# Storing both halves of the value product to DRAM and joining them on GpSimd by token group, in a fused attention and two-MLP kernel

## The chip, the cores and the metric

The kernel runs on one core of one Trainium2 chip. The metric is the device time of one execution in microseconds. A core has five engines that run their own instruction lists and meet only through semaphores: TensorE (PE, matrix products), VectorE (DVE), ScalarE (ACT), GpSimd (POOL) and SyncE (SP), which here issues every DMA. In the profile's rows "PEld" is TensorE loading the stationary operand, and "SPq" is the queue of SyncE.

## The reference

All inputs are float32. Three stages follow each other:

```python
def _attn_ref(q, k, v, s):                       # (4, 8, 576, 64); s is (4, 8, 576)
    scores = np.matmul(q, k.transpose(0, 1, 3, 2)) / np.sqrt(64)
    cum = np.cumsum(np.maximum(s, 0.0), axis=-1)
    bias = -(cum[:, :, :, None] - cum[:, :, None, :])
    scores = np.where(causal, -1e9, scores + np.minimum(bias, 0.0))
    attn = softmax(scores)
    return np.matmul(attn, v)
def _moe_ref(x, w_in, w_out, g_ln):              # x (2304, 512), hidden 1024
    h = x @ w_in
    solu = h * softmax(h)
    return (layer_norm(solu) * g_ln) @ w_out
def _moe2_ref(x, w1, w2, w3, w_out):             # hidden 768
    return np.maximum(np.maximum(x @ w1, x @ w2), x @ w3) @ w_out
```

The attention output of all 8 heads of a batch, side by side, is the row of 512 that enters the first MLP.

## The kernel before

**Precision.** Every product is made of float32 operands split in two: a high part that TensorE takes exactly, and a low part that holds the rest. A product is high times high plus the two mixed terms. In the value product the stationary operand `v_hl` (128 x 128) holds the high part of a head's v in columns 0 to 63 and the low part in columns 64 to 127. So the result in PSUM has 128 partitions for one head: partitions 0 to 63 are the product with the high half of v, partitions 64 to 127 that with the low half, and the two must be added to give the head's 64 output columns.

**Attention.** There are 32 heads (`HEADS`), worked on in slots. In slot t, TensorE (`slot`, L504) turns the probabilities of head t-1 (`turn`), computes the scores of head t, and does the value product of head t-2 (`values`) in two pieces: PV_A goes to PSUM bank 6 and PV_B to bank 7. The five engines each have their own slot function whose order is written out by hand, and each runs the steady slots two at a time in a loop (one turn is a pair, an even and an odd head), since all buffers come in twos.

- ACT (`slot`, L813 on): `pt_high` (copies turned probabilities, rounding them), `split_v`, five `exp`, and at the end of the slot `copy_vlo_a` and `copy_vlo_b`, which copy the low half (partitions 64 to 127) of banks 6 and 7 to SBUF.
- DVE: `q_low`, five `row_max`, four `pt_low`, and `add_a` and `add_b`, which add bank 6 or 7 (partitions 0 to 63) to the copied low half and write the result to `xT`, the attention output, that stays in SBUF.
- POOL: `qk_high` and `k_low` (the splits of q and k of head t+1: L670, L671, L672, L676), then `split_v` (L680, head t-1); in eight of the later pairs also a piece of the split of `w_in` (`split_win`, L691, L693).
- SP: `reload(t)`. All its waits stand in the queue, and everything behind a wait is held too:

```python
def reload(t, par, known=None):
    sp.wait_ge(k_hi_ready, t - 1); sp.wait_ge(q_lo_ready, t - 1); sp.wait_ge(k_lo_ready, t - 1)
    load_qk(t, par)
    if known != 2:
        sp.wait_ge(v_lo_ready, t - 2)
    load_v(t - 1, 1 - par)
    ...
    sp.wait_ge(scores_done, 3 * (t - 1))
    load_aux(t, par)
```

`load_qk` is two DMAs of 288 KB (L292), `load_v` two (L296, L297), `load_aux` one (L301). After every odd head of pairs 2 to 13 one piece of an MLP weight is loaded into `stage`: 512 KB of `w_in` in pairs 2 to 5 (L337), 256 KB of `w_out` in pairs 6 to 13 (L340).

**First MLP.** Tokens are taken in 6 groups of 384 (`GT`). For each group POOL's `divide(g)` (L723) multiplies a 128 x 1536 piece of `xT` by the reciprocals of the softmax sums, `rinvB`, which went through DRAM, and writes `xg`; ACT's `x_high` and DVE's `x_low` split it, and TensorE runs `hidden`, `turn_ln`, `second`. `divide(0)` stands in POOL's list between its slots 31 and 32, and ACT's first `x_high` stands before its slot 32, so the first group's input is prepared while the last heads are still in work. Later `divide`s stand ahead of the group before theirs. The second MLP follows.

## Time and profile before

| | |
|---|---|
| Median of 3 runs | 773.73 us (772.16 to 774.55) |
| Time of the profiled execution | 776.48 us |
| Span of the profiled execution, first to last instruction | 774.2 us |
| Busy share of the span | PE 93%, DVE 54%, ACT 42%, POOL 29% |
| Mean granted TensorE clock | 0.989 of full speed |
| DMA | 45.26 MB; HBM read 39.43 MB, written 5.38 MB |

The attention stage takes the first 240 us of the span. There all engines are busy; in the two MLPs behind it TensorE is busy nearly all the time and the others are not. Busy shares of a whole span are therefore no guide to a change in the attention stage: the rows further down are read stretch by stretch. A busy TensorE is a modelled figure, and an idle engine costs only where something waits for it.

### The profile page before, as it was taken

How to read it: one execution, taken by the hardware profiler on the slowest of the kernel's cores; microseconds unless marked ns; L12 is line 12 of the kernel's file. 1: busy time of each engine (PE TensorE's matmuls, PEld its weight loads, DVE VectorE, ACT ScalarE, POOL GpSimd, SP SyncE). 2: the span in 40 equal slices, each digit the busy share in tenths (PEclk: the TensorE clock that was granted, in tenths of full speed). 3: DMA queues.
4: the chain of work that ended last, by engine and by line, in shares of the span. 5: the costliest groups of instructions: out<-in, count | busy, mean ns of one | idle time of the engine just before them, and what ended most of it. 6: DMA issues, size and time to landing. Idle time of an engine off the chain costs nothing.

```text
span 774.2 us, 12663 instructions
## 1 busy us (share of the span) xinstructions
PE 720.6 (93%) x4248; PEld 664.9 (86%) x4248; DVE 418.0 (54%) x766; ACT 328.5 (42%) x795; POOL 226.3 (29%) x242
## 2 busy tenths in 40 slices
PE   2798898999889899999999999999999999999997
PEld 1787787888777788889898989999989999899995
DVE  8799999999995684635354463612313213132120
ACT  1688788888874443414232242412112112121111
POOL 6665768989742641304040200000000000000000
PEclk9799999999999999999999999999999999999999
DMA  6555455555341101105200022000010010000101
GB/s 136 118 140 153 130 144 131 141 133 137 95 91 42 42 13 29 42 1 145 60 0 0 0 81 83 1 14 28 1 41 1 1 40 1 30 11 0 41 0 41
DMA packets 46579, 45.26 MB, mean 58 GB/s; under 512 B 22164, under 2 KB 37652, under 8 KB 46516
## 3 DMA queue, kind: packets, MB, share of 16 engines
q1 hardware_dynamic: 46548, 44.86, 21.9%
q8 instruction: 18, 0.29, 0.2%
q14 instruction: 13, 0.11, 0.1%
HBM read 39.43 MB, written 5.38 MB: 58 GB/s over the span
## 4 chain that ended last, share of the span: by engine, by line
PE 65%; DVE 10%; DMA 7%; issue 6%; POOL 5%; SPq 4%; ACT 2%; DVEq 0%; POOLq 0%; ACTq 0%
PE ps L606 10%; PE ps L605 10%; PE ps L604 10%; DMA qk_raw<-in_qk_dram 7%; PE ps L536 4%; PE ps L538 4%; PE ps L537 4%; PE ps L524 3%; PE ps L526 3%; PE ps L525 3%; PE ps L617 3%; PE ps L619 3%; PE ps L618 3%; DVE nmax L1007 2%; POOL qk_b L676 2%
## 5 line engine op out<-in xcount | busy, mean ns | idle before, releaser
L606 PE MATMUL ps<-x_lo,w_hi 128*128 (+1 forms) x432 | 144.4, 334 | 0.0
L604 PE MATMUL ps<-x_hi,w_hi 128*128 128x384 f32 x432 | 144.3, 334 | 0.0
L605 PE MATMUL ps<-x_hi,w_lo 128*128 128x384 f32 x432 | 144.3, 334 | 0.0
L788 ACT ACTIVATE probs<-ps,nmax 128x576 f32<-128x576 f32 (+4 forms) x160 | 82.6, 530 | 17.2 <-DVE nmax L1007 17.2
L798 ACT ACTIVATE pt_hi<-ps 128x512 fp32r<-128x512 f32 (+1 forms) x128 | 69.8, 569 | 34.5 <-PE ps L433 28.3
L433 PE MATMUL ps<-ident,probs 128*128 128x128 f32 x480 | 74.3, 286 | 10.4 <-DVE pt_lo L1014 5.8
L440 PE MATMUL ps<-pt_hi,v_hl 128*128 128x256 f32 (+2 forms) x256 | 67.7, 294 | 16.5 <-DVE xT L1034 13.6
L604 PEld LDWEIGHTS ps<-x_hi,w_hi 128*128 128x128 f32 x432 | 81.1, 188 | 0.2
L605 PEld LDWEIGHTS ps<-x_hi,w_lo 128*128 128x128 f32 x432 | 81.1, 188 | 0.2
L606 PEld LDWEIGHTS ps<-x_lo,w_hi 128*128 128x128 f32 x432 | 81.1, 188 | 0.0
L1014 DVE TENSOR_TENSOR pt_lo<-ps,pt_hi 128x512 fp32r<-128x512 f32 (+1 forms) x128 | 78.0, 649 | 4.8 <-ACT pt_hi L798 3.9
L415 PE MATMUL ps<-k_a,q_a 128*128 128x288 f32 (+2 forms) x192 | 64.3, 342 | 14.5 <-DVE rinvT L1052 14.1
L1007 DVE TENSOR_REDUCE nmax<-ps 128x1 f32<-128x576 f32 (+4 forms) x160 | 72.7, 484 | 4.6 <-PE ps L420 3.2
L933 ACT ACTIVATE m_hi<-stage 128x384 fp32r<-128x384 f32 x36 | 18.9, 525 | 124.9 <-DVE stage L1193 124.9
L440 PEld LDWEIGHTS ps<-pt_hi,v_hl 128*128 128x128 f32 x256 | 49.3, 193 | 21.9 <-issue 14.3
L536 PE MATMUL ps<-lnT_hi,wout_hi 128*128 128x384 f32 x192 | 64.4, 335 | 2.7 <-DVE lnT_lo L1138 2.7
L433 PEld LDWEIGHTS ps<-ident,probs 128*128 128x128 f32 x480 | 53.3, 145 | 15.8 <-issue 6.9
L1195 DVE TENSOR_TENSOR m_lo<-stage,m_hi 128x384 fp32r<-128x384 f32 x36 | 20.1, 558 | 82.2 <-ACT m_hi L933 82.2
L538 PE MATMUL ps<-lnT_lo,wout_hi 128*128 128x384 f32 x192 | 64.2, 335 | 0.0
L537 PE MATMUL ps<-lnT_hi,wout_lo 128*128 128x384 f32 x192 | 64.2, 334 | 0.0
L441 PE MATMUL ps<-pt_lo,v_hl 128*128 128x256 f32 (+2 forms) x256 | 61.0, 286 | 0.0
L524 PE MATMUL ps<-win_hi,x_hi 128*128 128x512 f32 x144 | 57.5, 399 | 2.8 <-DVE ln L1122 2.1
(102 smaller groups left out, 1441.5 us busy)
## 6 DMA issues: line engine op xcount, KB each, us to landing
qk_raw<-in_qk_dram SPq DMA_DIRECT2D x64, 288.0 KB, 4.2
rinvB<-rsum_dram SPq DMA_DIRECT2D x24, 192.0 KB, 3.8
stage<-in_moe_w_dram SPq DMA_DIRECT2D x18, 256.0 KB, 4.4
out_dram<-stage SPq DMA_DIRECT2D x18, 256.0 KB, 2.0
v_raw<-in_v_dram SPq DMA_DIRECT2D x32, 128.0 KB, 2.4
stage<-in_moe_w_out_dram SPq DMA_DIRECT2D x14, 256.0 KB, 2.7
stage<-in_moe_w_in_dram SPq DMA_DIRECT2D x4, 512.0 KB, 3.6
aux_dram<-setup SPq DMA_DIRECT2D x1, 576.0 KB, 4.5
```

The costliest lines, as they stand in the source:

```text
L433: mm = pe.transpose(ps[:, GBANK[g], P * n:P * (n + 1)], probs[1 - par][:, o:o + P], ident[:, :])
L440: pe.matmul(dst, v_hl[par][:, j, :], pt_hi[par][:, a0:a1], start=(n == 0), stop=False)
L524: pe.matmul(dst, x_hi[ab][:, c, :], win_hi[:, c, cols], start=(c == 0), stop=False)
L536: pe.matmul(dst, wout_hi[:, f, cols], lnT_hi[:, f, :], start=(f == 0), stop=False)
L537: pe.matmul(dst, wout_lo[:, f, cols], lnT_hi[:, f, :], start=False, stop=False)
L538: mm = pe.matmul(dst, wout_hi[:, f, cols], lnT_lo[:, f, :], start=False, stop=(f == FB - 1))
L604: pe.matmul(dst, w_hi[f][:, i, c, :], x2_hi[par][:, c, :], start=(c == 0), stop=False)
L605: pe.matmul(dst, w_lo[f][:, i, c, :], x2_hi[par][:, c, :], start=False, stop=False)
L606: mm = pe.matmul(dst, w_hi[f][:, i, c, :], x2_lo[:, c, bass.ds(g * GT, GT)], start=False, stop=(c == KC - 1))
L788: act.activation(dst, SCORES[c], ACT.Exp, bias=nmax[par][:, c:c + 1], accum_out=sums_all[:, c, bass.ds(t, 1)]).then_inc(exp_done, 1)
L1007: dve.tensor_reduce(nmax[par][:, c:c + 1], SCORES[c], AX_XY if c == NCH - 1 else AX_X, ALU.max, negate=True).then_inc(max_done, 1)
L1014: dve.tensor_tensor(pt_lo[1 - par][:, o:o + n], ps[:, GBANK[g], 0:n], f32(pt_hi[1 - par][:, o:o + n]), ALU.subtract).then_inc(pt_lo_done, 1)
```

## The change

What the attention stage makes of a head's value product is changed:

- **Removed**: ACT's two copies of 64 partitions (`copy_vlo_a`, `copy_vlo_b`), and DVE's two adds (`add_a`, `add_b`) with the semaphores that TensorE, ACT and POOL wait on for them.
- **Added on ACT**: one copy of all 128 partitions of both banks (288 columns of each, 128 x 576) to one of two `halves` buffers.
- **Added on SP**: `store_x`, one DMA of 288 KB for each head, from `halves` to a DRAM tensor `x_dram` (head, partition, position). In the steady loop it stands behind `load_aux` in every `reload`, so ahead of the weight load and of the next head's q and k. `load_xa(b)` reads the high half of one batch (8 heads) back into `xT` with two DMAs of 576 KB; `load_xb(g)` reads the low half of one token group into a new buffer `xb` with four DMAs of 192 KB. The first of these stand among the last heads' reloads.
- **Added on POOL**: in each `divide(g)` an add of 128 x 1536, `xT` plus `xb`, ahead of the multiplication.
- **Moved**: the boundary between the pieces of the value product, so that each bank holds 288 columns. PV_A had pieces of 320, 256 and 128 columns and has 288, 224 and 96; PV_B had 4 of 256 and one of 128 and has 3 of 288, one of 256 and one of 128. The sum of columns and the number of matmuls stay.

```diff
-    PV_A = [(0, J0 + PAD, J0 + 3 * P, 0), (1, J1, J1 + 2 * P, PAD), (2, J2, J2 + P, PAD + P)]
+    PV_A = [(0, J0 + PAD, J0 + PAD + HALF, 0), (1, J1, J1 + HALF - PAD, PAD), (2, J2, J2 + HALF - P - PAD, P + PAD)]
...
+    x_dram = nc.dram_tensor("x_dram", (HEADS, P, S), F32, kind="Internal").ap()
...
@@ SP, reload @@
                 load_aux(t, par)
+                if known is None or known >= 5:
+                    store_x(t - 5, 1 - par)
+
+            def store_x(h, par):
+                sp.wait_ge(x_copied, h + 1)
+                rows = x_dram[bass.ds(h, 1)].rearrange("a p s -> (a p) s")
+                sp.dma_start(rows, halves[par][:, :, :].rearrange("p a b -> p (a b)")).then_inc(x_stored[par], 16)
+
+            def load_xa(b):
+                for par in range(2):
+                    sp.wait_ge(x_stored[par], 16 * (b + 1) * HB // 2)
+                for par in range(2):
+                    src = x_dram[HB * b:HB * (b + 1), 0:D, :].rearrange("(j r) d s -> r d j s", r=2)[par]
+                    sp.dma_start(xT[D * par:D * (par + 1), :, S * b:S * (b + 1)], src).then_inc(xa_loaded, 16)
...
@@ SP, last heads @@
             reload(HEADS - 4, 0)
+            load_xa(0)
             reload(HEADS - 3, 1)
+            load_xb(0)
             reload(HEADS - 2, 0)
+            load_xa(1)
             sp.wait_ge(rinv_done, 1)
...
@@ TensorE, slot @@
                     if known != 2:
-                        pe.wait_ge(xa_done, t - 2)
+                        pe.wait_ge(x_copied, t - 2)
                     values(t, par, 6, PV_A)
...
@@ POOL, divide @@
+                cols = xT[:, :, bass.ds(g * GT, GT)]
+                pool.wait_ge(xb_loaded, 64 * (g + 1))
+                pool.tensor_tensor(cols, cols, xb[:, :, :], ALU.add).then_inc(x_added, 1)
                 pool.wait_ge(rinvB_loaded, 64 * (g + 1))
                 if known != 0:
                     pool.wait_ge(x_lo_ready, 3 * g)
-                pool.tensor_tensor(xg[:, :, :], xT[:, :, bass.ds(g * GT, GT)], rinvB[:, :, :], ALU.mult).then_inc(xg_ready, 1)
+                pool.wait_ge(x_added, g + 1)
+                pool.tensor_tensor(xg[:, :, :], cols, rinvB[:, :, :], ALU.mult).then_inc(xg_ready, 1)
...
@@ ACT, end of a slot @@
-                act.activation(vlo_a[:, :], ps[D:P, 6, 0:QA], ACT.Copy).then_inc(vloa_copied, 1)
-                act.activation(vlo_b[:, :], ps[D:P, 7, 0:QB], ACT.Copy).then_inc(vlob_copied, 1)
+                if known is None or known >= 4:
+                    act.wait_ge(x_stored[par], (t - 2 - par) * 8)
+                act.wait_ge(pv_done, 2 * (t - 2) + 2)
+                act.activation(halves[par][:, :, :], ps[:, 6:8, 0:HALF], ACT.Copy).then_inc(x_copied, 1)
...
@@ DVE, slot @@
-                if live(known, 3):
-                    add_a(t, par, known)
...
-                if live(known, 3):
-                    add_b(t, par, known)
```

On SP, at the end of a turn of the loop over pairs 6 to 13, behind the odd head's `load_aux` (L301), the list changes so (in the rows "ISA" and REGISTER_ALU compute addresses and wait counts, and the next turn begins with the even head's `load_qk`):

```order
 L301 DMA qk_b1<-aux_dram 4x1152
-L340 ISA x2
-L340 DMA stage<-in_moe_w_out_dram 128x512
-L338 REGISTER_ALU
-L338 COMPARE_AND_BRANCH
+L331 REGISTER_ALU
+L333 ISA
+L333 DMA x_dram<-halves0 128x576
+L373 ISA x2
+L373 DMA stage<-in_moe_w_out_dram 128x512
+L371 REGISTER_ALU
+L371 COMPARE_AND_BRANCH
```

The store of a head now stands ahead of the weight load, and both stand ahead of the next pair's q and k.

On SP, at the reloads of heads 28 to 30, straight behind that loop (xT and xb are the buffers for the high and the low half):

```order
 L301 DMA qk_b0<-aux_dram 4x1152
+L333 DMA x_dram<-halves1 128x576
+L341 DMA xT<-x_dram 64x4x576 x2
 L292 DMA qk_raw1<-in_qk_dram 64x1152 x2
 L296 DMA v_raw0<-in_v_dram 64x64
 L297 DMA v_raw0<-in_v_dram 128x4x64
 L301 DMA qk_b1<-aux_dram 4x1152
+L333 DMA x_dram<-halves0 128x576
+L352 DMA xb<-x_dram 64x4x192 x4
 L292 DMA qk_raw0<-in_qk_dram 64x1152 x2
```

Ahead of head 29's q and k now stand a store and the read of a whole batch's high halves, and ahead of head 30's a store and four reads of low halves.

On POOL, where the attention stage hands over to the first MLP, the list of the changed kernel reads as follows (L722 is the split of v, L764 the add, L769 the multiplication that was L723, L795 the scaling of `w_out`):

```order
L764 TENSOR_TENSOR xT<-xT,xb 128x4x384
L769 TENSOR_TENSOR xg<-xT,rinvB 128x1536
L722 TENSOR_TENSOR v_hl<-v_raw,v_hl 128x5x64
L764 TENSOR_TENSOR xT<-xT,xb 128x4x384
L769 TENSOR_TENSOR xg<-xT,rinvB 128x1536
L795 TENSOR_SCALAR wout_hi<-stage,g_sb 128x512 x8
```

Each multiplication has an add ahead of it now; the order of the others has not moved.

## Rows read from the trace of the kernel before

**Rows 1.** Windows: busy us of each engine, then clock, DMA share, GB/s

```profile
40.00:60.00 20.00, 18.30 (x142) 16.68 (x141) 19.25 (x37) 17.73 (x53) 12.66 (x15) 1.00 0.60 159
160.00:180.00 20.00, 18.55 (x144) 16.85 (x142) 19.59 (x39) 17.61 (x53) 18.36 (x20) 1.00 0.52 138
```

**Rows 2.** Waits from 40 to 230 us: us in total, times, longest

```profile
POOL q_a L670 <- DMA qk_raw<-in_qk_dram: 25.5, 12, 3.9
...
PE ps L440 <- DVE xT L1034: 13.4, 21, 1.6
```

**Rows 3.** Groups by shape, 40 to 250 us: busy, mean ns, idle before

```profile
L788 ACT ACTIVATE probs<-ps,nmax 128x576 f32<-128x576 f32 x28 | 20.6, 735 | 1.0 <-DVE nmax L1007 1.0
...
L805 ACT ACTIVATE vlo_a<-ps 64x320 f32<-64x320 f32 x31 | 13.5, 434 | 6.8 <-PE ps L441 6.1
...
L1034 DVE TENSOR_TENSOR xT<-ps,vlo_a 64x320 f32 x24 | 11.6, 484 | 0.7
L812 ACT ACTIVATE vlo_b<-ps 64x256 f32<-64x256 f32 x31 | 11.5, 369 | 1.2 <-PE ps L441 1.2
...
L1041 DVE TENSOR_TENSOR xT<-ps,vlo_b 64x256 f32 x24 | 9.9, 413 | 0.4
```

**Rows 4.** Timeline of POOL in one pair: start us, us, what, idle before

```profile
130.66 0.67 POOL L670 TENSOR_SCALAR q_a<-qk_raw 128x576 fp32r<-128x576 f32 x1 [1.24 <-DMA qk_raw<-in_qk_dram]
...
132.57 1.92 POOL L676 TENSOR_TENSOR qk_b<-qk_raw,k_a 64x576 fp32r<-64x576 f32 x1
134.45 0.87 POOL L680 TENSOR_TENSOR v_hl<-v_raw,v_hl 128x320 fp32r<-128x320 f32 x1
...
143.74 0.67 POOL L670 TENSOR_SCALAR q_a<-qk_raw 128x576 fp32r<-128x576 f32 x1 [1.33 <-DMA qk_raw<-in_qk_dram]
```

**Rows 5.** Timeline of SP's queue in the same pair

```profile
135.49 0.47 SPq L296 DMA_DIRECT2D v_raw<-in_v_dram  x1
136.14 0.45 SPq L297 DMA_DIRECT2D v_raw<-in_v_dram  x1
136.84 0.27 SPq L301 DMA_DIRECT2D qk_b<-aux_dram  x1
137.43 0.36 SPq L340 DMA_DIRECT2D stage<-in_moe_w_out_dram  x1
138.49 1.18 SPq L292 DMA_DIRECT2D qk_raw<-in_qk_dram  x2
```

**Rows 6.** Chain in order of time: last q/k load of two pairs

```profile
85.58 5.29 DMA qk_raw<-in_qk_dram
...
139.20 4.28 DMA qk_raw<-in_qk_dram
```

**Rows 7.** Timeline of SP's queue, the pair that loads 512 KB

```profile
83.62 0.36 SPq L337 DMA_DIRECT2D stage<-in_moe_w_in_dram  x1
```

**Rows 8.** Timeline of POOL: splits of heads 4, 28, 29 and 30

```profile
32.92 0.67 POOL L670 TENSOR_SCALAR q_a<-qk_raw 128x576 fp32r<-128x576 f32 x1 [1.45 <-PE ps L420]
...
195.68 0.67 POOL L670 TENSOR_SCALAR q_a<-qk_raw 128x576 fp32r<-128x576 f32 x1 [0.95 <-DMA qk_raw<-in_qk_dram]
202.88 0.67 POOL L670 TENSOR_SCALAR q_a<-qk_raw 128x576 fp32r<-128x576 f32 x1
208.76 0.67 POOL L670 TENSOR_SCALAR q_a<-qk_raw 128x576 fp32r<-128x576 f32 x1 [0.43 <-PE ps L420]
```

**Rows 9.** Timeline of SP's queue: q and k of heads 29, 30

```profile
196.42 1.11 SPq L292 DMA_DIRECT2D qk_raw<-in_qk_dram  x2
...
202.15 1.11 SPq L292 DMA_DIRECT2D qk_raw<-in_qk_dram  x2
```

**Rows 10.** Waits of PE from 200 to 242 us

```profile
PE ps L440 <- DVE xT L1034: 2.8, 4, 1.5
```

**Rows 11.** Timeline of POOL and ACT at the hand-over

```profile
230.58 0.88 POOL L680 TENSOR_TENSOR v_hl<-v_raw,v_hl 128x320 fp32r<-128x320 f32 x1 [4.83 <-ACT v_hl L778]
231.41 3.49 POOL L723 TENSOR_TENSOR xg<-xT,rinvB 128x1536 f32<-128x1536 f32 x1
...
235.69 0.62 ACT L857 ACTIVATE x_hi<-xg 128x512 fp32r<-128x512 f32 x1
236.33 0.60 ACT L798 ACTIVATE pt_hi<-ps 128x512 fp32r<-128x512 f32 x1
```

**Rows 12.** Waits of POOL from 240 to 440 us

```profile
POOL xg L723 <- DVE x_lo L1091: 82.5, 5, 22.7
```

More of the change, by code:

```diff
@@ L124, in attention_and_mlp @@
             nmax = [sb(a, f"nmax{i}", [P, NCH]) for i in range(2)]
-            vlo_a = sb(a, "vlo_a", [D, QA])
-            vlo_b = sb(a, "vlo_b", [D, QB])
+            halves = [sb(a, f"halves{i}", [P, 2, HALF]) for i in range(2)]
             q_a = [sb(a, f"q_a{i}", [P, SP], F32R) for i in range(2)]
@@ L207, in attention_and_mlp @@
         pv_done = sem("pv_done")
-        vloa_copied = sem("vloa_copied")
-        vlob_copied = sem("vlob_copied")
-        xa_done = sem("xa_done")
-        xb_done = sem("xb_done")
+        x_copied = sem("x_copied")
+        x_stored = [sem(f"x_stored{i}") for i in range(2)]
+        xa_loaded = sem("xa_loaded")
+        xb_loaded = sem("xb_loaded")
+        x_added = sem("x_added")
         sums_turned = sem("sums_turned")
@@ L325, in reload, with load_xb, reload_pair, load_win @@
                 load_aux(t, par)
-            reload(2, 0, 2)
-            reload(3, 1)
-            def reload_pair(pair):
-                reload(2 * pair, 0)
-                reload(2 * pair + 1, 1)
-            with sp.Fori(2, 2 + KC) as pair:
+                if known is None or known >= 5:
[10 more added lines that the diff above has]
+                    sp.dma_start(xT[D * par:D * (par + 1), :, S * b:S * (b + 1)], src).then_inc(xa_loaded, 16)
+            def load_xb(g):
+                if g > 0:
+                    sp.wait_ge(x_added, g)
+                for part in range(2):
+                    b_, s0 = divmod(g * GT + part * GT // 2, S)
+                    for par in range(2):
+                        src = x_dram[HB * b_:HB * (b_ + 1), D:P, s0:s0 + GT // 2].rearrange("(j r) d t -> r d j t", r=2)[par]
+                        dst = xb[D * par:D * (par + 1), :, part * GT // 2:(part + 1) * GT // 2]
+                        sp.dma_start(dst, src).then_inc(xb_loaded, 16)
+            reload(2, 0, 2)
+            reload(3, 1, 3)
+            def reload_pair(pair, known=None):
+                reload(2 * pair, 0, known)
+                reload(2 * pair + 1, 1, known and known + 1)
+            def load_win(pair):
+                sp.dma_start(stage[:, bass.ds(pair * FF - 2 * FF, FF)], w_in[bass.ds(pair * P - 2 * P, P), :]).then_inc(w_loaded, 16)
+            reload_pair(2, 4)
+            load_win(2)
+            with sp.Fori(3, 2 + KC) as pair:
                 reload_pair(pair)
-                sp.dma_start(stage[:, bass.ds(pair * FF - 2 * FF, FF)], w_in[bass.ds(pair * P - 2 * P, P), :]).then_inc(w_loaded, 16)
+                load_win(pair)
             with sp.Fori(2 + KC, 2 + KC + FB) as pair:
@@ L377, in _ @@
                 load_rinv(g)
+                load_xb(g)
             def stage_block(f, slot):
@@ L573, in _ @@
             hidden(1, 1, 0)
-            pe.wait_ge(xa_done, HEADS)
-            pe.wait_ge(xb_done, HEADS)
+            pe.wait_ge(x_copied, HEADS)
             pe.wait_ge(rinvT_ready, 4)
@@ L1023, in invert_sums @@
                 dve.reciprocal(flat, flat).then_inc(rinv_done, 1)
-            def columns(t, par, known):
-                pair = (t - 4 + par) // 2 if known is not None else (t - 4 + par) >> 1
-                return (pair % KC) * TOKENS + (pair // KC) * S
-            def add_a(t, par, known):
-                flat = xT[:, :, :].rearrange("p c t -> p (c t)")
-                dve.wait_ge(vloa_copied, t - 2)
-                dve.tensor_tensor(flat[D * (1 - par):D * (2 - par), bass.ds(columns(t, par, known), QA)], ps[0:D, 6, 0:QA],
-                                  vlo_a[:, :], ALU.add).then_inc(xa_done, 1)
-            def add_b(t, par, known):
-                flat = xT[:, :, :].rearrange("p c t -> p (c t)")
-                dve.wait_ge(vlob_copied, t - 2)
-                dve.tensor_tensor(flat[D * (1 - par):D * (2 - par), bass.ds(columns(t, par, known) + QA, QB)], ps[0:D, 7, 0:QB],
-                                  vlo_b[:, :], ALU.add).then_inc(xb_done, 1)
             q_low(0, 0)
```

39 lines of the change are left out of this document (17 added, 22 removed).

## The prediction, written before the changed kernel was run

> **What bounds the kernel now.** I first read the windows of the attention stage. The reader is to see that DVE is busy 19.25 of 20 us early in the stage and 19.59 of 20 us later, ACT 17.7, TensorE 18.5 by its modelled figure [rows 1]. Taken alone that says DVE is the bound, and a change that takes work from DVE must win. The waits say something else beside it. TensorE waits 13.4 us in all, 21 times, for DVE's `add_a` before it may start PV_A. But POOL also waits 25.5 us, 12 times, for the q and k of the next head to land [rows 2]. Twelve is once in nearly every pair, always ahead of an even head.
>
> So I followed that wait around one pair in the timelines. POOL begins an even head's splits at 130.66 us, on the landing of the load. They and the split of v behind them end at 134.45 + 0.87 = 135.32 us [rows 4]. SP was waiting for exactly that: its next issue starts at 135.49, and it goes on without a gap through v, v, aux and the weight piece to the two q/k loads at 138.49 [rows 5]. The chain of waits then runs through the second of these loads, from 139.20 for 4.28 us, to 143.48 [rows 6], and POOL begins the next even head at 143.74, having sat idle for 1.33 us [rows 4]. This is a closed ring, POOL to SP to DMA to POOL, of 13.08 us, with no slack at any step, and it is as long as the pair. The kernel is thus held by two things at once: DVE's list (97% full) and this ring. Shortening the first gains nothing if the second gets longer.
>
> **The change part by part.**
>
> *DVE loses two adds*, 484 + 413 = 897 ns a head [rows 3], 1.8 us a pair. If DVE alone set the pace, 32 heads would gain up to 29 us. ACT and TensorE leave less room: ACT is busy 17.61 of 20 us, so at 88% of its present time it is full [rows 1]. What TensorE could get back is the 13.4 us it now waits for the adds [rows 2].
>
> *ACT* replaces copies of 434 + 369 = 803 ns [rows 3] by one of 128 x 576 from PSUM. The nearest row is the exponential of that shape, 735 ns [rows 3]. I take 735 ns, a gain of 0.07 us a slot that lies beside the ring: zero. The bounds are 0 and 2 us over the stage. The first copy could run while TensorE was still in PV_B and the new one can not, but ACT's next work needs TensorE's next transposes, so what is queued behind it would wait anyway.
>
> *TensorE* keeps its columns and its number of matmuls: zero. Its new wait at PV_A is for the copy at the end of the slot before, about 3 us earlier: zero. If that copy itself waits for the store that frees its buffer, everything moves; the store is issued one slot before the copy that needs the buffer, and I count 4 us between landing and need.
>
> *SP and the queue, 12 pairs.* From head 5 on each `reload` issues a store of 288 KB, behind aux and ahead of the weight load and q/k. For the ring this is the odd head's store: one store per turn. Its price is bounded from below by its issue alone. The v and aux issues follow each other by 0.65 to 0.70 us [rows 5], so 0.65 us. From above it is bounded by its bytes, since the queue drains in order. The trace has that experiment. With 256 KB of weights ahead of q/k, the time from the weight issue to the landing is 143.48 - 137.43 = 6.05 us [rows 5, 6]. With 512 KB it is 85.58 + 5.29 - 83.62 = 7.25 us [rows 6, 7]. So 256 KB more cost 1.20 us, and 288 KB would cost 1.35 us. The mean rate agrees roughly: 138 GB/s at a share of 0.52 is 265 GB/s when busy [rows 1], 1.1 us for the store. I take 1.2 us, between the two and near the measured one. The intervals it applies to are those between even heads 4 and 28, from 32.92 to 195.68 us [rows 8], 12 of them: 12 x 1.2 = **14.4 us** (7.8 to 16.2).
>
> The page "DMA: Bandwidth & Descriptors", section "Anatomy of one DMA", of the Trainium skill prices moving bytes at 436 GB/s on top of a fixed cost. By it the store would hold the queue 0.68 us, the issue would be its dearer part, and this term would be about 8 us instead of 14.4. The row with 256 KB more disagrees with the page by a factor of two, and I go by the row.
>
> *SP and the queue, last heads.* Ahead of head 29's q/k come a store and 1152 KB of high halves, ahead of head 30's a store and 768 KB of low halves: 2496 KB in all. Together with what stands there already (two times 576 KB, 144 and 18 KB) it is 3810 KB, 14.7 us at 265 GB/s. From the issue at 196.42 [rows 9] with about 1.5 us of latency this ends at 212.6 us. POOL began head 30 at 208.76, and it waited for TensorE there, not for DMA [rows 8]. That is 3.8 us late, and head 29 alone gives the same size: POOL began it without waiting at 202.88 [rows 8]. The two overlap. The read of batch 1 behind them runs while SP waits for the reciprocals anyway. I take **4 us** (0 if the queue's idle time takes it all; 8 if both add).
>
> *POOL's add at the hand-over.* `divide(0)` ran at 231.41 for 3.49 us, straight behind the split of v [rows 11]. The add has the same shape and two operands in SBUF: 3.49 us, ahead of it. ACT's first `x_high` at 235.69 needs the result, and ACT's last transposed probabilities at 236.33 are queued behind it [rows 11]. With `xg` at 238.4 instead of 234.9, ACT would start at about 238.5: **+2.7 us** (0 to 3.5), and TensorE's last slot and the first MLP tile wait for ACT. The five later adds (17.5 us of POOL) stand ahead of a wait of 82.5 us in five times that POOL has there [rows 12]: zero.
>
> *What the relief of DVE still gives.* Outside the 12 intervals, from 200 to 242 us, TensorE waits 2.8 us for the adds [rows 10]: **-2 us** (-3 to 0).
>
> The sum is 14.4 + 4 + 2.7 - 2 = **+19.1 us**. The profiled execution took 776.5 us, with 774.2 us of span; that becomes 795.6. The median of the runs shown is 2.8 us below the profiled one, so the time is 792.8, rounded 793 us.
>
> **The rivals.**
>
> *A, the relief wins (faster).* If the store's issue and bytes vanish in the ring's idle time, the pace is set by DVE, ACT and TensorE, and the 13.4 us of waits go, less 2.7 us at the hand-over: 773.7 - 10.7 = 763 us. Against it speaks that the ring has no idle step. It decides if the ring shortens by more than the 0.65 us that the issue alone costs. POOL's step is the one that could: `k_low` takes 1.92 us there [rows 4]. The page "SBUF — State Buffer" of the Trainium skill, section "Who interferes with whom", says that a DVE instruction with at most one SBUF input does not contend with GpSimd. The adds have one, so by that rule their removal leaves `k_low` as long as it is. Without that rule I would still doubt A, since the ring waits for DMA 1.33 us, not for POOL alone. Chance 0.17.
>
> *B, a draw.* The price is the bare issue, 7.8 us, the last heads' loads are hidden, and the relief gives back 8 to 10 us wherever the ring is not last. 774 us within 2. Chance 0.08.
>
> *C, the queue is worse (slower still).* The store's writes cost twice the 1.35 us, or the bulk reads add up to 8 us and TensorE's idle time brings its clock down. The clock is 1.00 in the stretches shown [rows 1], so a drop would be new. 14.4 doubles and 4 becomes 8: 773.7 + 37.5 = 811 us. Chance 0.13.
>
> *The forecast*, the ring grows by a store per turn: 0.62, its own range 779 to 802 (the sum with all lower bounds is 7.8 + 0 + 0 - 3 = +4.8; with all upper ones +27.7).
>
> **How the numbers follow.** Runs of this kernel can tell about 0.3%, 2.3 us, from no change. Faster: A, 0.17, and a little of B, 0.18. Same: 0.08. Slower: the forecast and C less what B takes, 0.74. The range leaves out half of A and the upper part of C: 765 to 804 us.
>
> **What the changed profile would show.** If I am right, the even heads' first split on POOL comes every 14.2 to 14.4 us where weight pieces of 256 KB are loaded, with idle time of 1.3 us or more ahead of it that ends on the q/k DMA. DVE's busy time falls from 19.6 to about 15.5 of 20 us. The wait of PV_A for DVE is gone, and TensorE waits for splits (`k_low`, `q_low`) or scores instead. The row of the store's issue is followed 0.65 us later by the weight issue, and the landing of the q/k loads is 7.2 us or more behind the store's issue. Around the reloads of heads 29 and 30 POOL waits 3 to 5 us for DMA. ACT sits idle about 2.7 us before its first `x_high`. If pairs take 13 us or less, the ring was not what I took it for and A holds. If ACT waits for the store to free `halves`, or TensorE for `x_copied`, I missed a wait.

## The result, and the profile after

The changed kernel takes 797.81 us (median of 4 runs, 793.96 to 800.65) against 773.69 us (4 runs, 772.16 to 774.55): ratio 1.0311, 95% interval 1.0264 to 1.0357. It is slower by 24 us, where the prediction said 19, in a range that holds it. A second comparison, on another chip, gave 794.67 against 774.44 us, ratio 1.0245 (1.0221 to 1.0268). The direction is sure; the size is between 19 and 24 us.

The profiled execution of the changed kernel took 800.65 us. The head of its page, for the busy shares, the granted clock in 40 slices, and the bytes:

```profile
span 798.9 us, 12576 instructions
...
PE 727.7 (91%) x4248; PEld 672.2 (84%) x4248; DVE 398.5 (50%) x702; ACT 325.1 (41%) x763; POOL 249.3 (31%) x248
...
PEclk9799999999987998999999999999999999999999
...
HBM read 48.87 MB, written 14.82 MB: 80 GB/s over the span
```

The reader is to see the low digits of the clock, 8 and 7 where the attention stage hands over to the first MLP (220 to 260 us) and 8 once more from 300 us, and 19 MB more of traffic. The windows of the attention stage, with the columns of [rows 1]:

```profile
40.00:60.00 20.00, 19.27 (x150) 17.37 (x149) 18.36 (x33) 18.16 (x54) 13.39 (x15) 1.00 0.68 196
160.00:180.00 20.00, 17.54 (x135) 15.89 (x134) 16.52 (x30) 16.95 (x47) 15.59 (x17) 1.00 0.64 173
```

From 160 to 180 us every engine is less busy than before: DVE has fallen from 19.59 to 16.52 us, TensorE from 18.55 to 17.54. Nobody is full any more; something that is no engine sets the pace. The waits from 40 to 250 us:

```profile
POOL q_a L712 <- DMA qk_raw<-in_qk_dram: 41.4, 14, 4.7
PEld ps L478 <- DVE pt_lo L1049: 38.4, 50, 5.0
DVE q_a L1035 <- POOL q_a L712: 31.8, 20, 5.9
```

TensorE's wait for the adds is gone, and POOL's wait for q and k has grown from 25.5 us in 12 times [rows 2] (the same 25.5 if its window too is taken to 250 us) to 41.4 in 14. DVE, which waited 2.7 us for POOL before, now waits 31.8. Its `pt_lo` stands behind that work in its list, so TensorE now waits for `pt_lo`: 30.8 us by its own row, 3.0 before. One turn of the ring, in SP's queue and on POOL (compare [rows 4, 5]):

```profile
139.11 0.47 SPq L296 DMA_DIRECT2D v_raw<-in_v_dram  x1
139.77 0.44 SPq L297 DMA_DIRECT2D v_raw<-in_v_dram  x1
140.48 0.27 SPq L301 DMA_DIRECT2D qk_b<-aux_dram  x1
141.00 0.36 SPq L333 DMA_DIRECT2D x_dram<-halves  x1
141.69 0.35 SPq L373 DMA_DIRECT2D stage<-in_moe_w_out_dram  x1
142.63 1.15 SPq L292 DMA_DIRECT2D qk_raw<-in_qk_dram  x2
```

```profile
134.29 0.67 POOL L712 TENSOR_SCALAR q_a<-qk_raw 128x576 fp32r<-128x576 f32 x1 [2.14 <-DMA qk_raw<-in_qk_dram]
...
138.08 0.87 POOL L722 TENSOR_TENSOR v_hl<-v_raw,v_hl 128x320 fp32r<-128x320 f32 x1
...
148.20 0.67 POOL L712 TENSOR_SCALAR q_a<-qk_raw 128x576 fp32r<-128x576 f32 x1 [2.17 <-DMA qk_raw<-in_qk_dram]
```

and the load in the chain of work that ended last:

```profile
143.24 4.69 DMA qk_raw<-in_qk_dram
```

The ring is closed as before, POOL to SP to DMA to POOL, and takes 148.20 - 134.29 = 13.91 us where it took 13.08. The 0.83 us come apart: from the first issue of v to the weight issue 2.58 us against 1.94, which is +0.64 us for one more issue, and from the weight issue to the landing of q and k 6.24 us against 6.05, +0.19. POOL's step is 4.82 against 4.83 us.

At the hand-over, POOL and ACT (compare [rows 11]):

```profile
244.11 0.88 POOL L722 TENSOR_TENSOR v_hl<-v_raw,v_hl 128x320 fp32r<-128x320 f32 x1 [6.60 <-ACT v_hl L821]
244.94 3.47 POOL L764 TENSOR_TENSOR xT<-xT,xb 128x1536 f32<-128x1536 f32 x1
248.56 3.43 POOL L769 TENSOR_TENSOR xg<-xT,rinvB 128x1536 f32<-128x1536 f32 x1
```

```profile
252.11 0.63 ACT L892 ACTIVATE x_hi<-xg 128x512 fp32r<-128x512 f32 x1 [3.46 <-POOL xg L769]
252.64 0.58 ACT L841 ACTIVATE pt_hi<-ps 128x512 fp32r<-128x512 f32 x1
```

To place the loss I cut the execution at five events that both kernels have: POOL's first split of heads 4, 28 and 31, the third and the sixth `x_low` of DVE (L1091 before, L1103 after), and the end of the span. Microseconds of each stretch:

| stretch | before | after | after, second comparison | cost |
|---|---|---|---|---|
| head 4 to head 28, 12 turns | 162.8 | 170.0 | 169.0 | +6.2 to 7.3 |
| head 28 to head 31 | 25.4 | 29.7 | 29.0 | +3.6 to 4.3 |
| head 31 to third `x_low` | 28.5 | 34.8 | 33.8 | +5.3 to 6.2 |
| third to sixth `x_low` | 33.9 | 37.6 | 37.4 | +3.5 to 3.7 |
| sixth `x_low` to the end | 490.7 | 493.6 | 492.7 | +2.0 to 2.9 |

With head 4 0.2 us later in the first run, and 0.7 us earlier in the second, the costs sum to 24.7 and 19.8 us of span. I read the stretches rather than the totals, and they repeat unequally. Each kernel has one trace, the changed one two. The fourth stretch repeats within 0.5 us over all kernels below with the same order, and the third within 0.1 us over the five that keep the hand-over of before. The first does not: two variants whose SP list is the changed kernel's up to head 28 took 168.2 and 172.3 us in it. Most of that scatter lies in its first four turns (58.7 to 61.7 us); the last eight took 109.0 to 110.8 us in these four traces, against 104.6 in the one trace of the kernel before. So the late turns are the safer measure of the ring: 0.55 to 0.78 us each. The end scatters by 1.8 us even where its code is unchanged (see the account further down).

The fourth stretch had no term in the prediction. DVE and POOL there:

```profile
285.91 0.68 DVE L1103 TENSOR_TENSOR x_lo<-xg,x_hi 128x512 fp32r<-128x512 f32 x1
287.31 0.15 DVE L1145 TENSOR_SCALAR stats<-stats 128x1 f32<-128x1 f32 x1 [0.71 <-ACT e L905]
287.38 9.35 DVE L1117 SCALAR_TENSOR_TENSOR wout_lo<-stage,g_sb,wout_hi 128x512 fp32r<-128x512 f32 x8
```

```profile
288.74 2.95 POOL L779 TENSOR_SCALAR ln<-ln,stats 128x1024 f32<-128x1024 f32 x1 [0.21 <-POOL stats L776]
291.65 3.87 POOL L764 TENSOR_TENSOR xT<-xT,xb 128x1536 f32<-128x1536 f32 x1
```

`wout_lo` is the split of the second weight of the first MLP, eight instructions of 128 x 512. It took 6.17 us in the trace of before and takes 9.35 us here, beside the third group's new add. The rows of its eight instructions (shortest, median and longest in ns), before and after, say how:

```profile
L1105 DVE SCALAR_TENSOR_TENSOR wout_lo<-stage,g_sb,wout_hi x8: 739/744/1530, 269.4 to 274.8; 128x512 fp32r<-128x512 f32 x8
L1117 DVE SCALAR_TENSOR_TENSOR wout_lo<-stage,g_sb,wout_hi x8: 741/742/3924, 287.4 to 296.0; 128x512 fp32r<-128x512 f32 x8
```

The eight are not all slower. The median is the same 0.74 us, and one of them takes 3.92 us, about as long as POOL's whole add.

### The profile page after: what moved, and what is told of

Its sections match the earlier page's. It is cut to its first block, busy times and chain, and to the rows that moved or that the text cites. A ratio compares the mean times of both kernels' runs of the same rounds, so it can differ in the third digit from the quotient of the medians.

```text
span 798.9 us, 12576 instructions
## 1 busy us (share of the span) xinstructions
PE 727.7 (91%) x4248; PEld 672.2 (84%) x4248; DVE 398.5 (50%) x702; ACT 325.1 (41%) x763; POOL 249.3 (31%) x248
## 4 chain that ended last, share of the span: by engine, by line
PE 65%; DMA 9%; POOL 7%; DVE 6%; issue 6%; SPq 5%; ACT 2%; POOLq 0%; DVEq 0%; ACTq 0%
PE ps L646 9%; PE ps L648 9%; PE ps L647 9%; DMA qk_raw<-in_qk_dram 9%; PE ps L579 4%; PE ps L581 4%; PE ps L580 4%; PE ps L567 3%; PE ps L568 3%; PE ps L569 3%; PE ps L659 3%; PE ps L661 3%; PE ps L660 3%; POOL qk_b L718 2%; PE ps L478 2%
## 5 line engine op out<-in xcount | busy, mean ns | idle before, releaser
L478 PE MATMUL ps<-ident,probs 128*128 128x128 f32 x480 | 80.0, 295 | 40.6 <-DVE pt_lo L1049 37.7
L478 PEld LDWEIGHTS ps<-ident,probs 128*128 128x128 f32 x480 | 55.0, 149 | 49.6 <-DVE pt_lo L1049 45.7
L1042 DVE TENSOR_REDUCE nmax<-ps 128x1 f32<-128x576 f32 (+4 forms) x160 | 69.7, 482 | 6.8 <-PE ps L465 5.7
L485 PE MATMUL ps<-pt_hi,v_hl 128*128 128x288 f32 (+4 forms) x256 | 70.7, 301 | 0.0
L486 PE MATMUL ps<-pt_lo,v_hl 128*128 128x288 f32 (+4 forms) x256 | 64.1, 296 | 0.0
L1035 DVE SCALAR_TENSOR_TENSOR q_a<-qk_raw,q_a 64x576 fp32r<-64x576 f32 x32 | 40.6, 1268 | 35.0 <-POOL q_a L712 34.7
```

What stands on the lines that cost most here:

```text
L478: mm = pe.transpose(ps[:, GBANK[g], P * n:P * (n + 1)], probs[1 - par][:, o:o + P], ident[:, :])
L485: pe.matmul(dst, v_hl[par][:, j, :], pt_hi[par][:, a0:a1], start=(n == 0), stop=False)
```

## The experiments

All ratios are to the kernel before on the same chip, with a 95% interval. The single moves were compared on other chips than the two results above, and the changed kernel's own ratio is 1.0311 or 1.0245. A variant's total is therefore weak evidence of what one move is worth; the stretches are better.

**Store behind q and k** (changed kernel; the store of a head comes one reload later, straight behind the issue of the next q and k):

```diff
                 load_qk(t, par)
+                if known is None or known >= 6:
+                    store_x(t - 6, par)
...
                 load_aux(t, par)
-                if known is None or known >= 5:
-                    store_x(t - 5, 1 - par)
```

> The changed kernel with each store issued one reload later, straight behind the load of q and k instead of ahead of the weight load and the next q and k. Same DMAs, same bytes. Theory R (the store's place in the ring POOL to SP to DMA to POOL is what costs): with 256 KB weight pieces the even heads' first split on POOL comes every 13.0 to 13.2 us again instead of 13.8 to 13.9, and the kernel gains 7 to 10 us on the changed one, to 788 to 791 us. Rival (the queue's bytes cost, wherever the store stands): the interval stays at 13.8 us and the time within 2 us of 798 us.

Measured: 787.23 us, ratio 1.0138 (1.0110 to 1.0167). Head 4 to head 28 took 164.8 us, so 5.2 of the 7.3 us came back. The late turns took 13.0 to 13.5 us (one 14.1), not 13.0 to 13.2 as expected. A new wait took some of it, since the buffer is now freed later (waits from 40 to 230 us):

```profile
ACT halves L849 <- DMA x_dram<-halves: 11.5, 6, 3.8
```

The store's place in SP's list is what cost the ring. This leaves open whether its issue or its bytes do.

**Few bytes, same issues** (changed kernel; leaves out of the stores all but 16 partitions, and the reads repeat stored rows, so the output isn't the reference's):

```diff
-                sp.dma_start(rows, halves[par][...]).then_inc(x_stored[par], 16)
+                sp.dma_start(rows[0:16, :], halves[par][0:16, ...]).then_inc(x_stored[par], 16)
```

> The changed kernel with stores of 16 partitions instead of 128 (36 KB instead of 288 KB), in the same place; the reads from DRAM keep their size but read rows that were stored, so the attention output is not the reference's. It splits the store's price in the ring into issue and bytes. If the issue on SP is the price (0.68 us between neighbours), the interval of even heads with 256 KB weights stays at 13.7 us, 0.1 below the changed kernel's, and the time falls by 2 us at most. If the bytes are the price as predicted (1.2 us or more), the interval returns to 13.1 to 13.3 us and the time falls by 6 to 8 us.

Measured: 796.76 us, ratio 1.0264 (1.0234 to 1.0294), no faster than the changed kernel. Late turns take 13.5 to 13.9 us, and the last eight sum to 110.8 us, as with full stores. An eighth of the store's bytes gives the same ring. So the store's bytes cost nothing that shows there, and what is left of the store is its issue.

**A store alone, in the kernel before** (a copy of 288 KB from `xT` to a spare DRAM tensor, in the place of `store_x`; first from head 5 on, then from head 6 on):

```diff
                 load_aux(t, par)
+                if known is None or known >= 6:      # 5 in the first version
+                    sp.wait_ge(xa_done, 2)
+                    sp.wait_ge(xb_done, 2)
+                    rows = x_dram[bass.ds(t - 5, 1)].rearrange("a p s -> (a p) s")
+                    sp.dma_start(rows, xT[:, 0, 0:S]).then_inc(x_stored, 16)
```

> The kernel before, its copies and adds on DVE kept, with one extra store of 288 KB per head from head 5 on, in the place where the changed kernel has it (the data stored are two heads' finished output, and nothing reads them). Theory R: the store alone costs 0.85 us or more in each of 12 even-to-even intervals, 10 to 16 us in all, so 784 to 790 us, and since DVE keeps its adds here the first four intervals, where DVE's relief hid it in the changed kernel, are longer too. Rival (the relief of DVE gave nothing, the ring alone counts): the same +7.5 us up to head 28 as in the changed kernel, so 781 us.

Measured: 790.38 us, ratio 1.0179 (1.0150 to 1.0207). This is not the price of a store. The turn from head 4 to head 6 alone took 21.5 us, since the first copy waited on SP for an add of a slot later; the late turns took 13.6 to 14.1. With the first copy moved by one head:

> The kernel before with an extra store of 288 KB per head in the changed kernel's place, from head 6 on. In the run of that kind from head 5 on, the first store waited for an add of one slot later, and the interval of heads 4 to 6 was 21.5 us; this one takes that wait out. Theory: with 256 KB weights each even-to-even interval is 13.75 us as there, 0.75 above the kernel before; the interval of heads 4 to 6 falls to 16 to 17 us; in all 8 to 11 us more than the kernel before up to head 28, and a ratio to it of 1.011 to 1.015. Then what DVE's relief gave back in the changed kernel's loop is 1 to 3 us. Rival: the ratio stays at 1.018, and the relief is worth 6 us or more.

Measured: 777.79 us, ratio 1.0077 (1.0046 to 1.0109). The last eight turns take 13.56 to 13.94 us, 109.9 in all against 104.6 in the kernel before: +0.67 us a turn (110.8 in the changed kernel). With ACT, DVE and POOL doing exactly their old work, the store alone makes the late turns of the changed kernel. So the longer turn there is no effect of the copies, the adds or the banks. In all it cost less than expected (a ratio of 1.011 to 1.015 was): the first four turns took 57.5 us, no more than before, and head 28 to head 31 23.0 us against 25.4, on which more below.

**A load in that place** (kernel before; 288 KB of q and k read into a spare buffer instead of the store, from head 5 on):

```diff
+                if known is None or known >= 5:
+                    if known != 5:
+                        sp.wait_ge(x_stored, 16 * (t - 5))
+                    sp.dma_start(spare_in[:, :], qkT[bass.ds(t - 5, 1)].rearrange("a d i s -> (a d i) s")).then_inc(x_stored, 16)
```

> The kernel before, with an extra load of 288 KB for each head from head 5 on (head t-5's q and k, 128 rows of 576, into a buffer nobody reads), in the place where the changed kernel has its store; all of the computation stays. Each load waits for the one before it, which was issued a slot earlier. The run with a store in that place gave intervals of mostly 13.5 to 13.9 us between even heads, h28 to h31 23.0 us, and a ratio of 1.0077. Theory 1, only the issue on SP counts (0.65 us), whichever way the bytes go: intervals of 13.6 to 13.9 us again, ratio 1.005 to 1.011. Theory 2, the bytes of a load compete with q and k and those of a store don't (the row of 512 KB against 256 KB of weights, 1.20 us for 256 KB, compared loads): 0.65 us for the issue and up to 1.35 us for the bytes, intervals of 14.2 to 14.8 us and a ratio of 1.014 to 1.025, with the landing of q and k 0.6 us or more farther behind their issue than in the run with the store.

Measured: 783.18 us, ratio 1.0086 (1.0064 to 1.0108), the ratio of the store within its interval. The last eight turns sum to 111.9 us, 0.24 a turn more than with a store, and one of them is 14.92. So in the late turns a load's bytes may cost a little, a fifth of the 1.35 us that my upper bound gave them. Theory 2 falls there. The first four turns, with weight pieces of 512 KB, took 61.1 us against 57.5 with a store; since the changed kernel's own scatter by 3 us, that settles nothing.

**Weight pieces behind the even head's q and k** (changed kernel):

```diff
-                reload_pair(pair)
-                load_wout(pair)
+                reload_pair(pair, None, lambda: load_wout(pair))   # issued behind load_qk of the even head
```

> The changed kernel with each weight piece loaded behind the even head's q and k instead of ahead of them; the stores stay in their place. Theory R (issues and bytes ahead of the even load set the ring): the ring loses a weight issue (0.63 to 0.95 us) and its bytes, so the even intervals fall from 13.8 to 12.7 to 13.1 us, and the 512 KB ones by more; 12 intervals give 9 to 14 us, a ratio of 1.013 to 1.020. Rival (with the adds gone another engine sets the pace at 13.8 us, or the odd ring becomes as long): the intervals stay at 13.5 us or more and the ratio at 1.027 to 1.031.

Measured: 782.29 us, ratio 1.0134 (1.0096 to 1.0171). The last eight turns take 12.6 to 13.2 us, all twelve 154.7 us: 15.3 us less than in the changed kernel and 8.1 less than before. SP's queue there, with nothing between the store and q and k:

```profile
135.02 0.28 SPq L301 DMA_DIRECT2D qk_b<-aux_dram  x1
135.56 0.37 SPq L335 DMA_DIRECT2D x_dram<-halves  x1
136.19 1.14 SPq L292 DMA_DIRECT2D qk_raw<-in_qk_dram  x2
```

**The same move in the kernel before:**

> The kernel before with the weight pieces loaded behind the even head's q and k, all else unchanged. It tells what held the kernel before at 13.0 us a pair. If both the ring and DVE's list, as I read the profile: the ring gets 0.8 us shorter, DVE's list at 97% allows 0.1 to 0.3 us of it in the later pairs and up to 0.8 us in the first ones, 2 to 6 us in all, a ratio of 0.992 to 0.997. Rival (the ring alone): 12.3 us a pair, 8 us or more, a ratio below 0.990.

Measured: 773.18 us, ratio 0.9979 (0.9961 to 0.9997). That is a little less than expected, and far from the rival. The twelve turns sum to 160.5 us against 162.8, but the gain lies in the first four; the last eight take 106.0 us, not less than the 104.6 of before. The window says what holds them:

```profile
100.00:120.00 20.00, 18.08 (x138) 16.27 (x138) 19.54 (x37) 17.73 (x53) 13.37 (x16) 1.00 0.52 127
```

DVE is busy 19.54 of 20 us. The two belong together: with the adds DVE's list holds the late turns at a mean of 13.1 us and more though the ring is shorter, without them the mean is 12.8, but only if the ring is shortened first. With the weights moved in both kernels, the change gains 160.5 - 154.7 = 5.8 us over the twelve turns in spite of its store, 106.0 - 102.6 = 3.4 of it in the last eight. This is the relief that rival A spoke of, and the change as made can't collect it.

**The bulk reads spread** (changed kernel; the reads of the first two batches and of the first group's low halves stand piece by piece behind the q and k of heads 20 to 25):

```diff
+            pieces = [lambda: load_xa(0, (0,)), lambda: load_xa(0, (1,)), lambda: load_xb(0, (0,)),
+                      lambda: load_xb(0, (1,)), lambda: load_xa(1, (0,)), lambda: load_xa(1, (1,))]
...
-            load_xa(0)
...
-            load_xb(0)
...
-            load_xa(1)
```

> The changed kernel with the reads of batches 0 and 1 (high halves) and of group 0 (low halves) taken out of the last heads' reloads and spread, one piece of 384 to 576 KB behind each load of q and k, over heads 20 to 25. Theory: heads 29 to 31 no longer wait for them; the stretch from head 28's split to head 31's falls from 29.7 us to about the 25.4 us of the kernel before plus a store or two, 26 us, and the kernel gains 3 to 5 us, a ratio to the kernel before of 1.025 to 1.027. Rival: they cost the same wherever they stand (the queue's bytes), heads 20 to 28 get longer by as much, and the ratio stays at 1.031.

Measured: 788.03 us, ratio 1.0196 (1.0155 to 1.0237). Head 28 to head 31 takes 22.4 us, 7.3 less than in the changed kernel and 3.0 less than before, and head 4 to head 28 took 168.7 us, no longer than the 169.0 and 170.0 of the changed kernel. So the rival falls: spread out behind the loads of q and k, the same bytes cost nothing that shows. The gain is more than the 3 to 5 us expected, since 25.4 us is no floor: with a store alone the kernel before takes 23.0 us there. Where the reads stood, SP's queue of the changed kernel reads:

```profile
203.23 0.35 SPq L333 DMA_DIRECT2D x_dram<-halves  x1
203.68 1.34 SPq L341 DMA_DIRECT2D xT<-x_dram  x2
205.13 1.19 SPq L292 DMA_DIRECT2D qk_raw<-in_qk_dram  x2
...
209.49 0.35 SPq L333 DMA_DIRECT2D x_dram<-halves  x1
209.88 2.61 SPq L352 DMA_DIRECT2D xb<-x_dram  x4
212.60 1.35 SPq L292 DMA_DIRECT2D qk_raw<-in_qk_dram  x2
```

and the chain has, for the load issued at 205.13:

```profile
205.72 9.02 DMA qk_raw<-in_qk_dram
```

The reads hold the queue by their issues (1.34 and 2.61 us), and here by their bytes too: this q and k took 9.02 us to land against 4.69 in the ring. 1152 KB directly ahead do what 288 KB two issues ahead do not. The read of batch 1 does the same to head 31. Its q and k, before and after:

```profile
216.11 1.12 SPq L292 DMA_DIRECT2D qk_raw<-in_qk_dram  x2
221.09 0.67 POOL L670 TENSOR_SCALAR q_a<-qk_raw 128x576 fp32r<-128x576 f32 x1 [1.29 <-DMA qk_raw<-in_qk_dram]
```

```profile
221.69 1.30 SPq L341 DMA_DIRECT2D xT<-x_dram  x2
225.34 1.13 SPq L292 DMA_DIRECT2D qk_raw<-in_qk_dram  x2
232.87 0.67 POOL L712 TENSOR_SCALAR q_a<-qk_raw 128x576 fp32r<-128x576 f32 x1 [3.27 <-DMA qk_raw<-in_qk_dram]
```

From the issue to POOL's split it is 5.0 us before and 7.5 us after.

**The first group's add one slot earlier on POOL** (changed kernel, ahead of its slot 31):

```diff
+            join(0)              # the wait for xb and the add
             slot(HEADS - 1, 1, HEADS - 1)
             divide(0, 0)         # now the multiplication alone
```

> The changed kernel with POOL's first add moved ahead of its slot 31, where it idles 6.6 us. Theory: ACT's idle time of 3.5 us before its first x_high is the add's, so the gap from the split of v of head 30 to x_high falls from 8.0 to 4.5 us, TensorE keeps its full clock at the first tile, and the kernel gains 3 to 5 us on the changed one, to 793 to 795 us. Rival (the data from DRAM come late there, not the add): the add waits for its loads in the new place, holds up the split of v of head 30, and the time stays within 1 us of 798 us.

Measured: 794.88 us, ratio 1.0240 (1.0212 to 1.0267). The total can't be told from the second comparison of the changed kernel. The stretch can: from head 31 to the third `x_low` 28.7 us, against 34.8 and 33.8 with the add in its place (32.5 to 33.8 in the other five variants that keep it there) and 28.5 before. The add at the hand-over costs 4 to 6 us, all of that stretch's loss but 0.2. TensorE's clock there did not stay full as expected: 0.91 from 236 to 256 us.

**The third group's add behind `wout_lo`** (changed kernel):

```diff
                 cols = xT[:, :, bass.ds(g * GT, GT)]
+                if isinstance(g, int) and g == 2:
+                    pool.wait_ge(wout_lo_ready, 1)
```

> The changed kernel with POOL's add for group 2 waiting until DVE has made wout_lo. Theory (an add on POOL and wout_lo on DVE, both with two operands in SBUF, hold each other up): DVE's wout_lo falls from 9.35 us back to 6.2 us, and the kernel gains 3 to 4 us, a ratio of 1.026 to 1.028. Rival: wout_lo is longer for another reason (the normalization at its side), stays above 9 us, and the ratio stays at 1.031.

Measured: 789.10 us, ratio 1.0207 (1.0168 to 1.0247). The split of the weight on DVE, and POOL's add behind it:

```profile
283.51 6.17 DVE L1119 SCALAR_TENSOR_TENSOR wout_lo<-stage,g_sb,wout_hi 128x512 fp32r<-128x512 f32 x8
```

```profile
289.84 3.46 POOL L766 TENSOR_TENSOR xT<-xT,xb 128x1536 f32<-128x1536 f32 x1 [2.02 <-DVE wout_lo L1119]
```

6.17 us again, and the add 3.46 us instead of 3.87. Third to sixth `x_low` takes 33.99 us, as before. In all seven kernels with the add beside `wout_lo` (both runs of the changed one and the five variants with that order) this stretch took 37.4 to 37.8 us; in the seven without the collision 33.8 to 34.0. The clock shows the rest of it; windows from 296 to 316 us, of the changed kernel and of this one:

```profile
296.00:316.00 20.00, 17.48 (x82) 16.19 (x83) 12.49 (x26) 8.01 (x14) 6.97 (x5) 0.83 0.24 54
```

```profile
296.00:316.00 20.00, 20.00 (x110) 18.99 (x109) 11.50 (x25) 7.59 (x13) 9.19 (x8) 1.00 0.36 79
```

**The changed kernel again**, for a closer interval and a second trace:

> The changed kernel itself, unchanged, on the chip of the two others and in more rounds, as the base for the differences: a ratio of 1.025 to 1.033. If it is below 1.025, the gains of the single moves are smaller than their differences to 1.0311 say.

Measured: 794.67 us, ratio 1.0245 (1.0221 to 1.0268), with the stretches shown in the table. It lies just below the 1.025 set beforehand, so the condition holds: by their ratios the single moves gain less than their differences to 1.0311 say. Against 1.0245 they are 8.6 us (weights), 3.8 (reads), 0.4 (first add) and 2.9 (third group's add).

**All four moves together** (changed kernel; weights behind q and k, reads spread, both adds moved; nothing left out):

> The changed kernel with four moves together, nothing left out: weight pieces behind the even head's q and k (alone it gave a ratio of 1.0134), the reads of batches 0 and 1 and of group 0's low halves spread over heads 20 to 25 (1.0196 alone), the first add ahead of POOL's slot 31 (1.024 alone), the add for group 2 behind wout_lo (1.0207 alone), against 1.0311 for the changed kernel. Theory: the costs are separate places on one chain, so the gains of 14, 7, 5 and 3 to 4 us add up to some 28 us and the kernel comes out faster than the one before, a ratio of 0.988 to 0.997. Rival (with the ring shortened, the next bound, DVE's and ACT's lists at 13 us a pair or the clock, takes the gains): 1.000 to 1.008.

Measured: 768.81 us (766.93 to 771.03), ratio 0.9922 (0.9901 to 0.9944). This version is 6 us (0.8%) faster than the kernel before and 26 us faster than the changed one. The four single gains sum to 16 us by the ratios and to 29 to 32 us by the stretches, so the stretches are the better account. Against the kernel before with its own weights moved, 773.18 us on the same chip, it is 4 us faster. From its page, the busy times and the clock:

```profile
PE 717.9 (93%) x4248; PEld 662.9 (86%) x4248; DVE 391.8 (51%) x702; ACT 323.1 (42%) x763; POOL 251.3 (33%) x248
...
PEclk9999999999999999999999999999999999999999
```

Head 31 is reached at 214.50 us (before 221.09), the next stretch takes 27.4 us and the one behind it 33.98.

## Why the prediction was right, and where it was not

The direction, the place of each cost at the ring, the last heads and the hand-over, and the range held; the total came out near by luck as well as by reason, since sizes were off both ways and one cost was missed. Terms in the order of the prediction, with the stretch that answers to each:

- **Two bounds at once, the ring and DVE's list.** Shown. The store alone, with DVE's work unchanged, makes the longer turn. Moving the weights gains 15.3 us over the twelve turns without the adds, 2.3 with them.
- **The ring, 14.4 us: mis-sized.** It cost 6.2 to 7.3 us over the twelve turns, 4.4 to 6.2 of it in the last eight. The step that failed is "I take 1.2 us, between the two and near the measured one": the turn grew by 0.83 us in the pair shown, 0.64 of it the issue, and by 0.67 with the store alone. The lower bound, the bare issue, was the right value. The row with 256 KB more priced another thing, a load directly ahead of q and k; the store stands two issues ahead. The first four turns were slow before the change already, 58.2 us in all, and took 1.0 us more, the last eight 6.2 us more. The estimate from the Trainium skill's page "DMA: Bandwidth & Descriptors", section "Anatomy of one DMA", was nearer in its result, about 8 us by its 436 GB/s against 14.4 by the row. That section gives the figure for DMAs issued from GpSimd, and here SP issues them. The estimate also makes the bytes (0.68 us) as dear as the issue (0.65), while the cut to an eighth of the bytes shows no byte term, so it came near by its total and not by its terms. Rival A's way out did not open either: POOL's step kept its length (`k_low` 1.41 us and the split ahead of it 1.18 in the pair shown, 1.92 and 0.66 before).
- **The last heads, 4 us: right as a sum**, 3.6 to 4.3, and partly by luck. The queue was late for heads 29, 30 and 31; POOL's waits for q and k there are 4.68, 2.84 and 3.27 us. But the prediction took batch 1's read as free beside SP's wait for the reciprocals, and it adds 2.5 us to head 31's load. On the other side the stretch of before had idle time in it: SP waited from 209.92 to 214.06 us for the reciprocals, ahead of head 31's load. The kernel before with a store is 2.6 us late at head 28 and only 0.2 at head 31. Measured from its 23.0 us the reads cost 6 to 7 us, and 4 is what is left of that. The 1.5 us of latency in the sum have no row; the shortest load of v took 1.8 us from issue to landing.
- **The add at the hand-over, 2.7 us: the place was right, the size half of what it is.** ACT sat idle 3.46 us, more than the 2.7 said. The stretch lost 5.3 to 6.2 us (4.0 at the least in the variants), above my upper bound of 3.5, and moving the add gave it back. What I had not priced is what follows the delay on TensorE. It waits over 4 us for DVE's `pt_lo` twice in this stretch and once ahead of it (4.92 us, in the last heads), and each time the next seven transposes take 1.75 us:

```profile
237.01 1.75 PE L478 MATMUL ps<-ident,probs 128*128 128x128 f32 x7 [4.44 <-DVE pt_lo L1049]
...
254.00 1.76 PE L478 MATMUL ps<-ident,probs 128*128 128x128 f32 x7 [4.10 <-DVE pt_lo L1049]
```

  Seven such transposes took 0.95 to 1.00 us in the trace of before, and 1.06 to 1.15 where no such wait stands ahead of them here. From 236 to 256 us the granted clock is 0.76; it was 1.00 from 230 to 250 before. The prediction had "TensorE's idle time brings its clock down" in rival C alone. That the clock turns 3.5 us of add into 5 to 6 us of stretch is my reading of these rows; no run separates the two.
- **The five later adds, zero: wrong for one of them.** I counted POOL's idle time and not what runs beside it. The third group's add delays DVE's `wout_lo` by 3.2 us, and TensorE waits for that: 3.5 to 3.7 us in the stretch. The Trainium skill, page "SBUF — State Buffer", section "Who interferes with whom", says that a DVE instruction with two SBUF inputs contends with a GpSimd instruction that reads SBUF. `wout_lo` has two, `stage` and `wout_hi`; the trace agrees, 9.35 us beside the add and 6.17 without, with one instruction of 3.92 us among seven short ones. I used the page's other half, on one input, and did not ask which DVE work the adds would newly stand beside.
- **The relief of DVE, -2 us: not seen** in its stretches, both of which got longer. With all four moves they take 22.7 and 27.4 us, 0.3 less than the kernel before with a store and 1.1 less than before, so about 1 us may be there; no run separates it.
- **The end, zero: +2.0 to 2.9 us**, in two parts. In the last 20 us of the span the first trace of the changed kernel has a granted clock of 0.91 (0.98 in the second), the kernel before 1.00. That part is no effect of the change: two variants of the kernel before (weights moved; store from head 5 on) have the same 0.91, and ends of 492.4 and 492.2 us against 490.6 to 490.7 in the other three. The other part, some 1.3 to 2.0 us, goes with the collision ahead of this stretch: in the 6 us ahead of the sixth `x_low` the clock is 0.59 and 0.50 in the two traces of the changed kernel, and what TensorE did not do there it does in this stretch. Where that clock was 0.94 or 1.00 (36 KB stores, weights moved, third group's add moved, all four), the end took 492.1 to 492.3 us, as in the two variants.
- **ACT, zero: right.** The copy of 128 x 576 took 653 ns where I took 735.

So an overpriced ring (7 to 8 us too much) stood against an underpriced hand-over, a missed collision and the end (8 to 10 us too little) and a relief of 2 us that did not come. Of what the changed profile was to show, right were: the store's issue followed 0.69 us later by the weight's (0.65 said), no wait of TensorE for adds, and no wait of ACT for `halves` or of TensorE for `x_copied`. Near were DVE's 16.5 us (15.5 said) and the landing 6.93 us behind the store's issue (7.2 or more said). Wrong were the turn, 13.9 instead of 14.2 to 14.4, and what TensorE waits for, `pt_lo` and not splits or scores. A small misreading: of the 12 waits for q and k [rows 2] eleven stand ahead of an even head, the twelfth ahead of head 31, the load behind the reciprocals.

Open: why the turns of heads 4 to 12 scatter (12.3 to 16.3 us over the kernels, without the 21.5 us above); and whether bytes of a store directly ahead of q and k would cost, which was not tried.

## What to carry to other kernels

In a closed ring through an in-order DMA issuer, first count the issues between the wait and the load that the ring needs. Here a store of 288 KB two issues ahead cost its issue and nothing more that shows, and moving the store or the weight load behind that load gave time back. Cut the bytes and keep the issues to tell the two apart. Work moved to an idle engine is not free because that engine waits: look at what the other engine runs at that moment, and at what TensorE's new idle time does to its granted clock.

## What the runs showed of the hardware

- In the turns shown the weight's issue followed the store's by 0.69 us, and the turn grew by 0.64 us of issue. The store's bytes, 288 or 36 KB, made no difference to the last eight turns (110.8 us both), and a load in its place made them 0.24 us longer each.
- In the late turns a load of q and k took 4.2 to 4.4 us before and 4.4 to 4.9 us in the two traces with a store two issues ahead (4.3 to 4.7 with 36 KB stores), but 9.02 us with 1152 KB directly ahead of it.
- After waits of 4.1 to 4.9 us TensorE ran seven transposes in 1.75 us instead of 1.0, and a window of 20 us came down to a granted clock of 0.76, between the levels of 1.2 and 2.4 GHz.
- A 3.5 us addition on GpSimd beside eight two-input DVE instructions cost DVE 3.2 us and GpSimd 0.4. One of the eight took 3.92 us, the median 0.74 as without it.
- In the last 20 us of the span the granted clock was 1.00 in some executions and 0.91 in others with the same code there, and the stretch was 1.5 to 1.8 us longer with 0.91.
